# Attention values in two passes with a high|low stationary operand, and the query placed by GpSimd

## The reference

```
attn:  scores = q k^T / 8, masked by blocks of 64 (a query block sees key blocks up to its own)
       attn_out = softmax(scores) v            4 batches x 8 heads, 576 tokens, head size 64
x = attn_out as (2304 tokens, 512)
moe:   out = sum over 4 experts of p_e * (relu(x w1_e) w2_e)          512 -> 1024 -> 512
moe2:  h = out w_in;  s = h * softmax(h);  result = layernorm(s) * g  w_out   512 -> 1024 -> 512
```

## Time and profile before

| what | value |
|---|---|
| median of 3 runs | 1188.47 us |
| profiled execution | 1189.02 us, span of the core 1187.2 us |
| granted TensorE clock, mean | 0.997 |
| TensorE products busy | 1164.0 us, 98% of the span, 6194 instructions |
| VectorE, ScalarE, GpSimd busy | 54%, 36%, 31% |
| attention | about 5.8 us to 229 us of the span |

### The profile page before, as it was taken

The page is one execution under the profiler, slowest core; times in us unless marked ns, Lnnn a source line. Parts: engine busy times, 40 slices in busy tenths (PEclk is TensorE's granted clock), DMA queues, the critical chain, the costliest instruction groups (busy, mean ns, idle before and its releaser), DMA issues.

```text
span 1187.2 us, 16802 instructions
## 1 busy us (share of the span) xinstructions
PE 1164.0 (98%) x6194; PEld 1041.6 (88%) x6194; DVE 635.4 (54%) x1155; ACT 428.0 (36%) x928; POOL 368.4 (31%) x333
## 2 busy tenths in 40 slices
PE   7999999999999999999999999999999999999997
PEld 6999999898999999999999999999999977888886
DVE  6887887654343533334443434452424478667764
ACT  6777787332322321113321112321112354433422
POOL 4676784252414300004400004410003453433320
PEclk9999999999999999999999999999999999999999
DMA  6777774665582404071504043513125100000000
GB/s 164 175 192 194 184 193 129 261 234 213 181 291 76 175 3 184 1 257 55 204 1 186 1 174 102 185 55 114 73 83 192 54 1 9 28 19 27 18 27 36
DMA packets 98740, 140.97 MB, mean 119 GB/s; under 512 B 40816, under 2 KB 69488, under 8 KB 98544
## 3 DMA queue, kind: packets, MB, share of 16 engines
q1 hardware_dynamic: 98672, 140.06, 36.4%
HBM read 105.16 MB, written 26.03 MB: 110 GB/s over the span
## 4 chain that ended last, share of the span: by engine, by line
PE 91%; ACT 3%; DVE 3%; issue 1%; POOL 1%; DMA 0%; SPq 0%; DVEq 0%; ACTq 0%; POOLq 0%
PE s L1649 36%; PE outp L1517 26%; PE s L1517 14%; PE ring L1517 11%; PE ring L1528 3%; ACT ptr_h L856 1%; PE ring L1778 1%; ACT pr L851 1%; DVE ptr_l L1146 1%; PE s L1721 1%; DVE ln_l L1411 0%; DMA q_over<-in_q 0%; DVE ex L1423 0%; ACT y_t L1045 0%; POOL y_s L790 0%
## 5 line engine op out<-in xcount | busy, mean ns | idle before, releaser
L1649 PE MATMUL s<-xr,w1s 128*128 128x384 f32 x2016 | 358.5, 336 | 0.4 <-DVE u L1353 0.4
L1649 PEld LDWEIGHTS s<-xr,w1s 128*128 128x128 f32 x2016 | 350.7, 188 | 4.4 <-DVE u L1353 0.7
L998 ACT ACTIVATE hid_h<-u 128x384 fp32r<-128x384 f32 x96 | 50.4, 525 | 371.7 <-DVE u L1348 346.2
L710 POOL TENSOR_TENSOR sums<-stage 128x256 f32<-128x256 f32 x20 | 14.7, 734 | 392.5 <-DMA stage<-in_moe_w 266.9
L1303 DVE SCALAR_TENSOR_TENSOR hid_l<-s,hid_h 128x384 fp32r<-128x384 f32 x48 | 26.7, 557 | 126.3 <-ACT hid_h L994 126.3
L1649 PE MATMUL s<-w1s,yop_h 128*128 128x512 f32 x252 | 86.3, 400 | 3.6 <-DVE h_b L1392 1.9
L1517 PE MATMUL s<-k_h,qb 128*128 128x288 f32 (+8 forms) x320 | 75.8, 326 | 8.0 <-DVE qb L1226 5.8
L851 ACT ACTIVATE pr<-s,neg_max 128x576 f32<-128x576 f32 (+2 forms) x144 | 74.8, 524 | 20.5 <-DVE neg_max L1139 17.1
L1263 DVE TENSOR_TENSOR u<-s,m_b 128x384 f32<-128x384 f32 x24 | 13.4, 558 | 128.2 <-PE s L1649 128.2
L994 ACT ACTIVATE hid_h<-s 128x384 fp32r<-128x384 f32 x48 | 23.6, 491 | 155.8 <-PE s L1517 155.4
L1517 PE MATMUL outp<-w_h,hid_h 128*128 128x512 f32 x192 | 75.5, 393 | 0.0
(11 more groups left out here) (168 smaller groups left out, 2452.8 us busy)
## 6 DMA issues: line engine op xcount, KB each, us to landing
xr<-x_stash SPq DMA_DIRECT2D x77, 768.0 KB, 6.2
stage<-in_moe_w SPq DMA_DIRECT2D x64, 256.0 KB, 5.1
x_stash<-x_tmp SPq DMA_DIRECT2D x12, 768.0 KB, 4.1
qb<-q_hl SPq DMA_DIRECT2D x30, 288.0 KB, 5.4
x_stash<-xr SPq DMA_DIRECT2D x1, 5376.0 KB, 16.9
k_raw<-in_k SPq DMA_DIRECT2D x16, 288.0 KB, 3.3
q_over<-in_q SPq DMA_DIRECT2D x16, 288.0 KB, 4.0
r_sb<-r_scratch SPq DMA_DIRECT2D x32, 144.0 KB, 3.2
```

The costliest lines, as they stand in the source:

```text
L710: pool.tensor_tensor(s1, a21, a22, ALU.add).then_inc(w1_sums, 1)
L998: act.activation(hid[slot][0][:, :], source, ACT.Relu).then_inc(hid_high, 1)
L1649: last = pe.matmul(target, x, y, start=start and i == 0, stop=stop and i == 2, skip_group_check=True)
```

## The change

The values are multiplied in two passes: the stationary operand is v's high part beside its low part (`v_hl`, 64 + 64 columns, one head), the moving operand the high part of the probabilities, then the low part. The upper 64 rows of the output are the high part's sum, the lower 64 the low part's (this includes low x low, which three passes leave out). The two halves are stored apart (`x_rows` has twice the rows), and GpSimd adds them when x is loaded back (`x_join`). Blocks 4 to 8 are now right (one head to a bank), blocks 0 to 3 left. The turns are regrouped. The query is split and placed by GpSimd in four instructions of 64 partitions (`split_query`), and the placing DMAs go. `x_n` is doubled, its store stands before `spread_r`, and `x_add` and the rounds of x are reordered, so that x's casts and low parts stand in pairs 11 to 14.

```diff
-             ((4, 2), (5, 2), (0, 0), (1, 0)),
-             ((2, 0), (3, 0), (2, 1), (3, 1))]
+             ((4, 2), (5, 2), (2, 1), (3, 1)),
+             ((0, 0), (1, 0), (2, 0), (3, 0))]
-    ROUNDS = [(B11,), (B21, B22), (T1, T2), (T3, T4)]
+    ROUNDS = [(B21, B22), (B11, T3), (T1, T2), (T4,)]
...
+            def both(target, a, b, start, stop):
+                pe.matmul(target, a, b[0], start=start, stop=False)
+                return pe.matmul(target, a, b[1], start=False, stop=stop)
...
+            def values_right(p, h, j0, j1):
...
                 for j in range(j0, j1):
+                    n = R_BLOCKS - (0, 0, 0, 2, 4)[j]
+                    end = 512 * h + R_WIDE
+                    last = both(outp[:, end - n * BLOCK:end].rearrange("p (b x) -> p b x", b=n), v_of(j, h),
+                                (right_part(0, j, h), right_part(1, j, h)), j == 0, j == KC - 1)
...
 SP, for each p
                 if p + 2 < PAIRS:
                     load_k(p + 2)
-                    place_q(p + 2)
                 store_r(p)
                 if p + 1 < PAIRS:
                     load_v(p + 1)
-                spread_r(p)
                 if p >= 1:
                     store_x(p - 1)
-                if p + 4 < PAIRS:
-                    load_q(p + 4)
+                spread_r(p)
+                if p + 3 < PAIRS:
+                    load_q(p + 3)
...
-                if p == 11:
+                if p == 12:
                     load_x(0, 1)
...
 GpSimd
+            def split_query(p):
+                pool.wait_ge(q_loaded[p % 2], 16 * (p // 2 + 1))
...
+                for h in range(2):
+                    pool.tensor_copy(placed[0][h], raw[h]).then_inc(q_high, 1)
+                pool.wait_ge(q_high, 2 * p)
+                pool.tensor_tensor(placed[1][0], raw[0], placed[0][0].bitcast(f32), ALU.subtract)
+                pool.tensor_tensor(placed[1][1], raw[1], placed[0][1].bitcast(f32), ALU.subtract).then_inc(q_split, 1)
...
+            def x_join(sg, t):
+                i = 2 * sg + t
+                pool.wait_ge(x_loaded, 64 * (i + 1))
...
+                pool.tensor_tensor(x_source(sg)[0], x_top, x_bottom, ALU.add).then_inc(x_added, 1)
...
 ScalarE
-                if r < 2:
-                    act.wait_ge(x_loaded, 32 * (i + 1))
+                if r == 0:
+                    act.wait_ge(x_added, i + 1)
                 else:
-                    act.wait_ge(x_sums, 3 * i + r)
+                    act.wait_ge(x_sums, 4 * i + r + 1)
```

More of the change, by code:

```diff
@@ L918, in late, with step @@
                     w1_cast_sums(0, p // 2 - 1)
-            def step(p, par, first=False, scores=True, ahead=True):
+            def step(p, par, ahead=True):
                 n = p + 1
@@ L984, in _ @@
                 exp_scores(b, 0)
-            step(0, 0, first=True)
-            for p in range(1, PAIRS - 1):
+            for p in range(PAIRS - 1):
                 step(p, p % 2, ahead=p < PAIRS - 2)
@@ L1181, in step, with scale_right @@
-            def step(p, par, first=False, scores=True, ahead=True):
+                dve.tensor_tensor(two_heads(x_n[par])[:, :, 0:L_WIDE],
+                                  outp[:, 0:2 * L_WIDE].rearrange("p (h x) -> p h x", h=2),
+                                  two_heads(r_sb)[:, :, 0:L_WIDE], ALU.mult).then_inc(left_scaled, 1)
+            def scale_right(p, par, h):
+                dve.wait_ge(r_loaded, 16 * (p + 1))
+                dve.wait_ge(right_done, 2 * p + h + 1)
+                if not (isinstance(p, int) and p < 2):
+                    dve.wait_ge(x_stored, 32 * (p - 1))
+                cols = slice(h * SEQ + L_WIDE, (h + 1) * SEQ)
+                dve.tensor_tensor(x_n[par][:, cols], outp[:, 512 * h:512 * h + R_WIDE], r_sb[:, cols], ALU.mult
+                                  ).then_inc(right_scaled, 1)
@@ L1182, in step @@
+            def step(p, par, first=False, ahead=True):
                 n = p + 1
                 if not first:
-                    scale_right(p - 1)
+                    scale_right(p - 1, 1 - par, 0)
                 floor_sums(p)
+                invert_sums(p)
+                max_scores(8, n)
+                low(T8, p, par)
                 if not first:
-                    scale_left(p - 1)
-                invert_sums(p)
-                if scores:
-                    max_scores(8, n)
@@ L1588, in values_right, with all_right @@
+                for j in range(j0, j1):
+                    n = R_BLOCKS - (0, 0, 0, 2, 4)[j]
+                    end = 512 * h + R_WIDE
+                    last = both(outp[:, end - n * BLOCK:end].rearrange("p (b x) -> p b x", b=n), v_of(j, h),
+                                (right_part(0, j, h), right_part(1, j, h)), j == 0, j == KC - 1)
                 if j1 == KC:
                     last.then_inc(right_done, 1)
+            def all_right(p):
+                for j0, j1 in ((0, 2), (2, KC)):
+                    for h in range(2):
+                        values_right(p, h, j0, j1)
@@ L1603, in step, with last_step @@
                 scores(2, n, slot)
+                turn(T67B, p, par)
+                scores(3, n, slot)
+                turn(T45, p, par)
+                scores(4, n, slot)
+                turn(T452, p, par)
+                scores(5, n, slot)
+                turn(T0123, p, par)
+                all_right(p)
+            def last_step(p, par):
+                turn(T8, p, par)
+                values_left(p - 1)
+                turn(T8R, p, par)
+                up(0, "m1")
                 turn(T67, p, par)
```

489 lines of the change are left out of this document (230 added, 259 removed).

## The result

The changed kernel takes 1219.05 us (median of 4 runs, 1217.91 to 1224.6) against 1188.47 before (4 runs too): ratio 1.0267, 95% interval 1.024 to 1.0293. It is slower by 30.6 us, where 1181 was forecast, and outside the range of 1170 to 1195.

What follows compares the result with a forecast made beforehand. TensorE was taken to bound the kernel. Products -20, start -2, pair 13 +8.8, slow clock +1.0 and first expert +4.3 sum to -7.9 us: from 1189.02 to 1181.1, median forecast 1181 us, range 1170 to 1195.

Steps and rivals of the forecast that it cites:

- The products: Value products in each attention pair: 5.04 us become 3.60; with 0.2 kept back, 1.25 us a pair, 20 us in all.
- The cover of VectorE and GpSimd: In plain pairs both engines follow the shorter period of 11.4 us, VectorE busy 10.7; costed at nothing.
- Doubled DMAs: Spread of r and store of x add 0.6 MB a pair: costs nothing, up to 0.6 us a pair if late.
- the walk: Step-by-step timing of the new attention pair from the previous pair's last transposes: left values to 5.0, end at 11.4 us.
- The other pairs with work on x: Attention pairs besides pair 13: GpSimd's added work on w1 or x fits the period; costed at nothing.
- Pair 13: Late x load, GpSimd's sum and ScalarE's casts delay pair 15's scores: loss 8.8 us (5 to 13), plus 1.0 slow clock.
- rival 1: GpSimd's half-height instructions run one after the other, pair 13 loses 13.2 us: about 1187 us in all; chance 0.22.
- First expert: Behind attention, x's later load, sum and cast delay the second unit by 3.0 us, then 1.3 more: 4.3 (0 to 9).
- Start: At the kernel's start the wait for the block-diagonal DMA goes: 2 us gained (0.5 to 3.5).
- rival 4: VectorE or the late r sets the attention pace, 12.0 us a pair, saving halved to 11 us: 1190 us; chance 0.08.
- Rival 2: GpSimd becomes attention's bound, from 7.2 us a pair for values and query, with serial halves and dear copies: 1195; chance 0.12.
- Rival 3: The loads of x stay hidden, landing earlier without the 256-byte pieces in the queues: 1170 us; chance 0.16.

Runs made afterwards that it cites:

- e2: The changed kernel with the spread of r issued ahead of the load of v and both stores of x: 1196.65 us.
- e9: e8 with the load of the next group of x moved from pair 14 to pair 15, behind the store of x, ahead of the stash: 1184.24 us.
- e12: e9 with joins in quarters, differences behind query 15, and low parts on GpSimd and casts on ScalarE moved to later pairs: 1182.06 us.
- e5: e2 with the second x tile's load earlier: lower half at the end of pair 11, upper half behind pair 12's spread of r: 1190.07 us.
- e8: e5 with the first two differences ahead of query 15, and the next group of x loaded in pair 14 and joined earlier: 1188.13 us.

## Why the prediction was wrong

- **The products: right.** The value products of the pair shown take 2.66 us (48.80 to 51.46) and 0.98 (54.91 to 55.89) in the kernel after, 3.64 together, where 3.60 were priced. Pairs 1 to 10 take 103.3 us in e2, 1.25 us a pair less than before, the figure of the sum; that the 0.2 us kept back were just what was lost is luck. The cover of VectorE and GpSimd in a plain pair, costed at nothing, held.
- **Doubled DMAs: the step that failed.** "r is issued at 9.8, lands near 13.8 and is due at 15: nothing, and up to 0.6 us a pair if it is late." It cost 22.4 us (e2 against after). What was wrong is the landing: the four microseconds were right for 576 KB first in line (e2: 4.0), and wrong behind the load of v and the 576 KB of stores that the change had put ahead of it (6.6). The time of issue was right: the store of r follows the left products, which end at 5.0 in the walk, by 0.9 us in the trace, and the spread follows it by 4.1, which makes 10.0 for 9.8. With 6.6 us from there r is 1.6 us late by the forecast's own walk; TensorE waited 1.9 in each of 12 pairs. The walk had reckoned with the late place (r first in line goes out 1.5 us behind its store) and found it free. Its own sign was a plain period over 11.8 us; it was 13.66. I had walked the engines to a tenth of a microsecond and the queue with one number.
- **The other pairs with work on x: not free.** "The other pairs I cost at nothing." In e2, where r is in time, pairs 10 to 13 take 36.5 us, and three periods of 11.48 are 34.4. TensorE waits 2.04 us for the low part of the key, which VectorE made under the join of pair 10 (140.34 to 143.80) in 3.58 us, where its median is 0.76:

```profile
140.83 3.58 DVE L1167 SCALAR_TENSOR_TENSOR k_l<-k_raw,k_h 128x576 fp32r<-128x576 f32 x1 [0.38 <-ACT k_h L884]
```

- **Pair 13: mechanism right, price small.** Forecast 8.8 and 1.0 for the clock; measured, pairs 13 to 15 take 13.1 us more than before, 15.6 with the 2.5 that their shorter products should have saved. Part of the difference is rival 1: the halves of a query are serial. In that case I had asked for 13.2 and 2 for the clock, which is close. The load was slower too: 9.6 us from the first issue to the join, where 8 were allowed.
- **First expert: mechanism right, price half.** Forecast 4.3; measured 8.6, and 9.8 with the last pair's saving. The load was issued from 246.5 us and landed at 259.5, 13 us later; I had allowed it 12 (223.6 to 235.6). TensorE waited 4.8 us where 3.0 were forecast for the second unit. In the 100 us behind the copy of pair 15 it was busy 91.49 us, before 98.19: 6.7 of the 9.8 us are time without work. The rest fits the lower clock (granted 0.97 in this stretch, before 1.00), for which the forecast had no term here. In e9, with the load ahead of the stash, the span behind pair 15 is 3.4 us shorter; the 5.2 us that it still has over the kernel before came back in no run.
- **Start: open.** 1.4 us by the table, but the same start took 26.8 to 31.3 us in the twelve experiments, so that the forecast's 2 us is neither shown nor refuted.
- **The rivals.** Rival 1 was the right one on GpSimd, and at 1187 still 32 us short, for the late r was in none but rival 4, which had it ("VectorE or the late r") at 12.0 a pair; it was 13.66. Rival 2's bound, 7.2 us, was not reached in a plain pair: copies took 0.69, so values and query are 6.6 us. In pairs 11 to 14, with the joins, GpSimd was at its bound or near it (e12: busy 45.3 us of the 45.9 that four short periods have). Rival 3's loads were not hidden.

By the rule of the Trainium skill on independent cores (GPSIMD Engine Reference, section 2.1) two half-height instructions would overlap; here the second starts as the first ends, 1.45 to 1.49 us behind its start in all 15 queries. The measurement decides.

## To carry to other kernels

Price a DMA at its place in the queue, bytes ahead of it and the waits of its neighbours included, and check the slack of each small transfer on the path before moving a large one past it: here one line moved back was worth 20 of the 31 us. A wait removed by moving work to another place in the same engine's order must be followed to where it comes out next (e5, e8, e12). A long instruction on GpSimd is also a risk for VectorE's short ones.

## What the runs showed of the hardware

- Two of VectorE's instructions did not get done before the running GpSimd instruction had ended. The floor of nine sums a partition took 3.44 us under a join that started 0.02 us ahead of it (e8) and 0.17 when it came 0.02 us first (e9); the low part of the key took 3.58 for 0.76 (e2). That both operands lie in SBUF is not enough for it: the reciprocal of the same nine sums took 0.22 us inside the join of e9 (172.08 to 175.59):

```profile
172.27 0.22 DVE L1188 RECIPROCAL rinv_wide<-sums_e 128x9 f32<-128x9 f32 x1
```

Between e8 and e9, whose orders up to there are the same, 0.04 us decided which came first, and TensorE waited 2.6 us in e8 and not in e9. The Trainium skill (SBUF — State Buffer, two separate sides) calls the port pair that VectorE and GpSimd share an exclusive lock, which whichever starts first gets for the whole instruction, for some forms of VectorE's instructions. The trace agrees, and the prediction had seen it for one short instruction and had not asked what the new long ones would do.
- The time from issue to landing of the same 576 KB was 4.0 to 6.6 us by what stood ahead in SyncE's queue; half the bytes in the same place gained 0.1 to 0.9 us.
- The lower level of TensorE's clock followed its waits: the granted clock was 0.69 from 264 to 275 us of the kernel after, so for a part of it at the lower level (1.2 GHz), a stretch with a wait of 4.8 us, in which TensorE was busy 6.84 of 11 us; in the first expert of the kernel before, with no wait in the stretch, it is 1.00.
